# Attention, routed experts and a gated MLP in one kernel: turns moved among products, a last step in halves, register reads moved

## The chip, the cores and the metric

One core of one Trainium2 chip runs the whole program. The metric is the device time of one execution in microseconds, lower is better; the times shown are medians over several executions.

## The reference

Three stages over 3072 tokens of 512 features, all fp32:

```
y[:, t] = scale * q_t @ state_t,  state_t = gamma * state_{t-1} + k_t v_t^T      # linear attention, 4 x 8 heads of 64
e = argmax(x @ w_gate);  h = relu(x @ w1[e]);  out = gate_w * sigmoid(x @ w_output_gate)[e] * (h @ w2[e])   # 8 experts, 512 -> 1024 -> 512
xn = x / rms(x) * rms_g;  g = xn @ w_gate;  result = (g * sigmoid(g) * (xn @ w_val)) @ w_out                 # MLP, 512 -> 1536 -> 512
```

## The kernel before, in words

Every engine has its own program, written out by hand, and they meet in counting semaphores: `then_inc` at the end of an instruction, `wait_ge` in front of one. Nothing plans the order; it is the order of the calls. In loops over tiles and blocks a wait compares with a value computed from the loop's counter in the engine's registers.

Large products run in three parts: an operand is split into a high part (`...h`, fp32r, written by ScalarE) and a low part (`...l`, the rest, by VectorE), and high times high, high times low and low times high are summed in one bank of 128x512. So every weight and every activation passes ScalarE first and VectorE second.

Stage 1, attention: 24 units of 128 tokens. Each unit's rows are scattered by an indirect DMA to the rows of their expert.

Stage 2, experts: tiles of 128 rows of one expert. Tiles 0 and 1 (`LEAD`) are written out; 2 to 21 run in a loop, 22 and 23 (`SURE - 2`, `SURE - 1`) are written out since the first work for the MLP lies around them, and from 24 (`SURE`) on, loops run a tile where a flag `real` in memory says that it exists; with this data tiles 24 to 28 do. On TensorE a tile `a` (`expert_tile`) is: `up(a, at, 0)` and `up(a, at, 1)`, 12 products each, with a half of the hidden row block each; `turn_hidden`, four turns (transposes through TensorE) of the first half of `hid`, then `turn_rows(a + 1)`, four turns of the next tile's rows `xg`, then four of the second half of `hid`; `down_tile`, 24 products. ScalarE: `tile_result` of the tile before, then three copies of weights where the next expert's are being split (`EARLY`, `HELD_EARLY`), `relu` of half 0, the store of the result, `relu` of half 1, `turned_hi_parts` (`hidh` half 0, `xgh` of the next tile by `rows_hi`, `hidh` half 1) and one more copy of weights. VectorE follows with `w1l`/`w2l`, `hidl`, `xgl`, `hidl`. Each expert's weights are 8 pieces of 128x1024; one tile splits the four of w1, the next the four of w2. GpSimd fetches the next tile's rows by an indirect DMA into `xg` once `tile_turned` says that it is free. The turned halves of `hid` go to banks HT0 and HT1, the rows to XG_T.

Stage 3, MLP: 6 blocks of 512 tokens, 12 inner steps of 128 hidden columns each (`NF`). On TensorE a step is `gate_value(n, f)`, 24 products in two banks, then `down(n, f - 1)`, 12 products into four sums; `down(n, 11)` ends the block. Between them for each step: `gate_sigmoid` (ScalarE, `sig`), `gated` and `prod` (`hidden`, VectorE), `hidden_hi` (ScalarE, `hh`), `hidden_lo` (VectorE, `hl`), each one instruction on 128x512. Behind step 11 ScalarE and VectorE make the next block's `xh` and `xl` (`turned_hi`, `turned_lo`). For blocks 0 and 1 the normalised rows are turned by TensorE (`turn_xn`): for block 0 around tile 23, eight turns before it and eight behind it, for block 1 inside block 0's last step; for the later blocks by DMAs and VectorE. In front of block 0 TensorE reads `runs` and `extra` from memory (`value_load`), and `real` flags one by one.

## Time and profile before

| what | value |
|---|---|
| median of 3 executions | 1116.9 us (1116.73 to 1118.97) |
| the profiled execution | 1117.19 us, span of its instructions 1115.4 us |
| TensorE busy (PE), weight loads (PEld) | 1093.2 us (98%), 908.0 us (81%) |
| VectorE (DVE), ScalarE (ACT), GpSimd (POOL) | 441.2 us (40%), 377.8 us (34%), 176.9 us (16%) |
| chain of waits that ended last | PE 92%, DVE 3%, DMA 2%, issue 2%, ACT 1% |
| granted TensorE clock | 1.0 over the span |
| stages | attention to about 145 us, experts to about 515 us, MLP to the end |

Busy time counts an instruction from its start to its end; products of TensorE overlap, so 0.389 us of one product's duration stands for a pitch of 0.227 us from start to start. "issue" as a releaser means that the engine waited for nothing that the profile shows. Line numbers are those of the kernel before.

### The profile page before, as it was taken

Reading aid. Unit: us, or ns where it says so; the run is one execution under the profiler, and the core shown is the slowest. Engines: PE = TensorE matmul, PEld = TensorE weight load, DVE = VectorE, ACT = ScalarE, POOL = GpSimd, SP = SyncE. Lnnn points to the kernel's source line nnn. Section 1 sums busy time; section 2 is a strip of 40 time slices with the busy share of each in tenths; the row PEclk is TensorE's granted clock in tenths of the full one; section 3 lists DMA queues with packets and bytes.
Section 4 is the critical chain, followed back from the end, with each engine's and each line's share of the span. In section 5 each row is a group of like instructions: output and inputs, shape, how many; then the busy total and the mean of one; then the engine's idle time right before and its main releaser. Section 6 shows DMA issues by size and latency. Waiting matters only on the chain.

```text
span 1115.4 us, 20314 instructions
## 1 busy us (share of the span) xinstructions
PE 1093.2 (98%) x6307; PEld 908.0 (81%) x6308; DVE 441.2 (40%) x868; ACT 377.8 (34%) x613; POOL 176.9 (16%) x245
## 2 busy tenths in 40 slices
PE   7999999999999999999999999999999999999998
PEld 6888888888888888787888888788878878887886
DVE  4777767332414425432433333423333242333222
ACT  3545435343525446432224231231133122212112
POOL 2444423322221201000000300200030011001000
PEclk9999999999999999999999999999999999999999
DMA  9999816434445533422201210111021001101001
GB/s 216 243 252 240 245 61 211 148 113 122 113 122 168 172 122 133 153 76 97 63 6 34 76 35 4 47 28 38 0 75 26 12 38 38 38 0 38 1 1 38
DMA packets 114068, 101.52 MB, mean 91 GB/s; under 512 B 81856, under 2 KB 87392, under 8 KB 114016
## 3 DMA queue, kind: packets, MB, share of 16 engines
q1 hardware_dynamic: 98752, 66.07, 22.2%
q0 software_dynamic: 8832, 26.81, 7.7%
q10 hardware_dynamic: 6432, 7.96, 2.0%
q8 instruction: 31, 0.51, 0.2%
q14 instruction: 21, 0.17, 0.1%
HBM read 76.41 MB, written 20.22 MB: 87 GB/s over the span
## 4 chain that ended last, share of the span: by engine, by line
PE 92%; DVE 3%; DMA 2%; issue 2%; ACT 1%; POOL 0%; SPq 0%; POOLq 0%; ACTq 0%; DVEq 0%
PE bank L720 14%; PE bank L722 14%; PE bank L721 14%; PE banks L644 14%; PE bank L617 14%; PE banks L720 3%; PE banks L722 3%; PE banks L721 3%; PE bank L528 2%; PE banks L514 2%; PE bank L558 1%; DMA x_rows<-x_out,slot_idx 1%; PE banks L632 1%; PE bank L608 1%; PE bank L632 1%
## 5 line engine op out<-in xcount | busy, mean ns | idle before, releaser
L1397 DVE TENSOR_TENSOR gated<-bank,sig 128x512 f32<-128x512 f32 x72 | 49.8, 692 | 344.1 <-ACT sig L1011 344.1
L1011 ACT ACTIVATE sig<-bank 128x512 f32<-128x512 f32 x72 | 43.1, 598 | 328.9 <-PE bank L722 328.9
L720 PE MATMUL bank<-xh,w1h 128*128 128x512 f32 x384 | 149.4, 389 | 0.0
L721 PE MATMUL bank<-xl,w1h 128*128 128x512 f32 x384 | 149.4, 389 | 0.0
L722 PE MATMUL bank<-xh,w1l 128*128 128x512 f32 x384 | 149.4, 389 | 0.0
L721 PEld LDWEIGHTS bank<-xl,w1h 128*128 128x128 f32 x384 | 72.1, 188 | 15.0
L722 PEld LDWEIGHTS bank<-xh,w1l 128*128 128x128 f32 x384 | 72.1, 188 | 15.0
L720 PEld LDWEIGHTS bank<-xh,w1h 128*128 128x128 f32 x384 | 72.1, 188 | 14.9
L1018 ACT ACTIVATE hh<-prod 128x512 fp32r<-128x512 f32 x72 | 45.5, 632 | 110.7 <-DVE prod L1401 110.7
L1163 DVE TENSOR_TENSOR hidl<-bank,hidh 128x512 fp32r<-128x512 f32 x29 | 20.0, 691 | 131.8 <-ACT hidh L869 131.8
L1406 DVE TENSOR_TENSOR hl<-prod,hh 128x512 fp32r<-128x512 f32 x72 | 49.9, 692 | 54.2 <-ACT hh L1018 54.2
L1598 POOL DMA_INDIRECT out_rows<-x_out,cur_idx x10 | 10.1, 1007 | 380.4 <-ACT x_out L1025 290.0
L644 PE MATMUL banks<-w2h,hidh 128*128 (+1 forms) x232 | 64.8, 401 | 0.4
L617 PE MATMUL bank<-w1h,xgh 128*128 (+1 forms) x232 | 62.7, 392 | 1.3 <-issue 1.3
L1128 DVE TENSOR_TENSOR w1l<-stage,w1h 128x1024 f32 (+1 forms) x40 | 48.1, 1232 | 39.7 <-ACT w1h L821 39.7
L644 PE MATMUL banks<-w2h,hidl 128*128 (+1 forms) x232 | 62.2, 390 | 0.0
L644 PE MATMUL banks<-w2l,hidh 128*128 (+1 forms) x232 | 62.2, 390 | 0.0
L617 PE MATMUL bank<-w1h,xgl 128*128 (+1 forms) x232 | 62.2, 390 | 0.0
L617 PE MATMUL bank<-w1l,xgh 128*128 (+1 forms) x232 | 62.0, 389 | 0.0
L852 ACT ACTIVATE hid<-bank 128x512 f32<-128x512 f32 x58 | 34.4, 594 | 79.9 <-PE bank L617 79.9
L1503 POOL DMA_INDIRECT xg<-x_rows,cur_idx x28 | 28.6, 1022 | 206.4 <-PE bank L608 204.7
L720 PE MATMUL banks<-w2h,hh 128*128 128x512 f32 x144 | 56.8, 394 | 4.4 <-DVE hl L1406 4.4
(243 smaller groups left out, 2130.6 us busy)
## 6 DMA issues: line engine op xcount, KB each, us to landing
stage<-in_moe_w SPq DMA_DIRECT2D x64, 512.0 KB, 5.6
expert_rows<-tile_o ACTq DMA_DIRECT2D x29, 256.0 KB
q_raw<-in_q SPq DMA_DIRECT2D x24, 256.0 KB, 6.0
k_raw<-in_k SPq DMA_DIRECT2D x24, 256.0 KB, 6.5
v_raw<-in_v SPq DMA_DIRECT2D x24, 256.0 KB, 4.6
stage<-stage SPq DMA_DIRECT2D x64, 64.0 KB, 2.0
stage<-in_moe_w_out SPq DMA_DIRECT2D x6, 512.0 KB, 4.1
stage<-in_moe_w_gate SPq DMA_DIRECT2D x5, 512.0 KB, 5.4
```

The source lines that it names most:

```text
L617: mm = pe.matmul(bank[(UP0, UP1)[g]][:, :], x[:, i, :], wt[:, ds(at + (i * FE + g * 512), 512)], start=(n == 0), stop=(n == len(terms) - 1))
L644: mm = pe.matmul(bank[DOWN][:, :], x[:, f, :], wt[:, ds(at + f * D, D)], start=(f == 0 and x is hidh and wt is w2h), stop=(f == KE - 1 and ...
L720: pe.matmul(out_ap, lh, rh, start=first, stop=False)
L721: pe.matmul(out_ap, lh, rl, start=False, stop=False)
L722: return pe.matmul(out_ap, ll, rh, start=False, stop=last)
L852: nc.scalar.activation(hid[:, g * 512:(g + 1) * 512], bank[(UP0, UP1)[g]][:, :], ACT.Relu)\
L1011: nc.scalar.activation(sig[:], bank[GV[f % 2][0]][:, :], ACT.Sigmoid).then_inc(s["sig_done"], 1)
L1018: nc.scalar.activation(hh[:, f % 2, :], prod[:], ACT.Copy).then_inc(s["hid_hi"], 1)
L1128: nc.vector.tensor_tensor(into[:, ds(at, PIECE)], stage[:, i % STAGE, :], hi[:, ds(at, PIECE)].bitcast(F32), ALU.subtract).then_inc(s["lo_ ...
L1397: v3.tensor_tensor(gated[:], bank[GV[f % 2][0]][:, :], sig[:], ALU.mult).then_inc(s["gated_done"], 1)
L1406: v3.tensor_tensor(hl[:, f % 2, :], prod[:], hh[:, f % 2, :].bitcast(F32), ALU.subtract)\
L1503: nc.gpsimd.indirect_dma_start(xg[:].bitcast(U32), None, x_dram, bass.IndirectOffsetOnAxis(cur_idx[:, 0:1], 0))\
```

## The change

The change has six parts.

- A tile's turns on TensorE: `turn_hidden(a, 0)` stands in the middle of `up(a, at, 1)`, behind six of its products (`between`); `turn_hidden(a, 1)` in `down_tile`, behind the first four products; `turn_rows(a + 1)` between the two halves of `down_tile`.
- ScalarE and VectorE follow that order: `hidh` half 0, `relu` half 1, `hidh` half 1, `xgh`; `hidl`, `hidl`, `xgl`.
- Step 11 of each MLP block runs on VectorE as gate(0), product(0), gate(1), hl(0), product(1), hl(1), each on 256 of the 512 tokens, on ScalarE as one sigmoid and two copies for `hh`. A block counts 13 in the semaphores of these (`STEPS`). `down(n, 11)` waits for the second half before its third sum.
- TensorE's reads of `runs`, `extra` and `real[LIKELY]` move to places around tiles 22 and 23.
- `hidden_hi` waits for `down_done` before `prod_done`; it was the other way round.
- In block 0 the first products into bank XG_T wait for `tileT_lo` of the last tile.

```diff
 F2 = 1536
 NF = F2 // P
+STEPS = NF + 1
...
+        def halves(f):
+            return range(2 if f == NF - 1 else 1)
+
+        def step_no(n, f, half=0):
+            return STEPS * n + f + half
+
+        def tokens_of(f, half):
+            return slice(half * 2 * P, (half + 1) * 2 * P) if f == NF - 1 else slice(0, BLK * P)
...
-            def up(a, at, g):
+            def up(a, at, g, between=None):
                 if not (isinstance(a, int) and a == 0):
                     pe.wait_ge(s["relu_done"], 2 * a - 1 + g)
                 terms = [(x, wt, i) for x, wt in ((xgh, w1h), (xgh, w1l), (xgl, w1h)) for i in range(KD)]
                 for n, (x, wt, i) in enumerate(terms):
+                    if between and n == len(terms) // 2:
+                        between()
                     mm = pe.matmul(bank[(UP0, UP1)[g]][:, :], x[:, i, :], wt[:, ds(at + (i * FE + g * 512), 512)],
                                    start=(n == 0), stop=(n == len(terms) - 1))
                 mm.then_inc(s["up_done"], 1)
-            def turn_hidden(a):
-
-                first = isinstance(a, int) and a == 0
+            def turn_hidden(a, g):
+
+                pe.wait_ge(s["relu_done"], 2 * a + g + 1)
+                if not (isinstance(a, int) and a == 0):
+                    pe.wait_ge(s["hTl"], 2 * a - 1 + g)
+                for i in range(4):
+                    f = 4 * g + i
+                    mm = pe.transpose(quad((HT0, HT1)[g])[:, i, :], hid[:, f * P:(f + 1) * P], ident)
+                mm.then_inc(s["h_turned"], 1)
+
+            def down_tile(a, at):
+
+                if not (isinstance(a, int) and a == 0):
+                    pe.wait_ge(s["tile_out"], a)
                 for g in range(2):
                     if g:
                         turn_rows(a + 1)
-                    pe.wait_ge(s["relu_done"], 2 * a + g + 1)
-                    if not first:
-                        pe.wait_ge(s["hTl"], 2 * a - 1 + g)
-                    for i in range(4):
-                        f = 4 * g + i
-                        mm = pe.transpose(quad((HT0, HT1)[g])[:, i, :], hid[:, f * P:(f + 1) * P], ident)
-                    mm.then_inc(s["h_turned"], 1)
-
-            def down_tile(a, at):
-
-                if not (isinstance(a, int) and a == 0):
-                    pe.wait_ge(s["tile_out"], a)
-                for g in range(2):
                     for x, wt in ((hidh, w2h), (hidh, w2l), (hidl, w2h)):
+                        if not g and x is hidh and wt is w2l:
+                            turn_hidden(a, 1)
                         if wt is w2h:
                             pe.wait_ge(s["hTh" if x is hidh else "hTl"], 2 * a + g + 1)
                         for f in range(4 * g, 4 * g + 4):
...
                 run = pe.value_load(run_of[0:1, ds(a, 1)], min_val=0, max_val=EXPERTS - 1)
                 pe.wait_ge(s["tileT_lo"], a + 1)
                 pe.wait_ge(s["lo_done"], RUN * run + PER)
-                for g in range(2):
-                    up(a, at, g)
-                turn_hidden(a)
+                up(a, at, 0)
+                up(a, at, 1, lambda: turn_hidden(a, 0))
                 pe.wait_ge(s["lo_done"], RUN * run + RUN)
                 down_tile(a, at)
...
             gate_logits(last)
             pe.wait_ge(s["x_out"], last)
             turn_x(last)
-            up(0, 0, 1)
+            up(0, 0, 1, lambda: turn_hidden(0, 0))
             ranks(last)
-            turn_hidden(0)
             pe.wait_ge(s["xT_out"], UNITS)
             down_tile(0, 0)
             for a in range(1, LEAD):
                 pe.wait_ge(s["tileT_lo"], a + 1)
-                for g in range(2):
-                    up(a, 0, g)
-                turn_hidden(a)
+                up(a, 0, 0)
+                up(a, 0, 1, lambda: turn_hidden(a, 0))
                 down_tile(a, 0)
             def turn_xn(n, halves):
...
             pe.wait_ge(s["control_ready"], 1)
             with pe.Fori(LEAD, SURE - 2) as a:
                 expert_tile(a)
+            runs = pe.value_load(flags[0:1, 0:1], min_val=0, max_val=EXPERTS - 2) + 2
             expert_tile(SURE - 2)
+            extra = pe.value_load(flags[0:1, 2:3], min_val=0, max_val=TILES - SURE)
             turn_xn(0, [0])
+            unlikely = pe.value_load(real[0:1, LIKELY:LIKELY + 1], min_val=0, max_val=1)
             expert_tile(SURE - 1)
             pe.wait_ge(s["xl_ready"], 2)
             turn_xn(0, [1])
-            runs = pe.value_load(flags[0:1, 0:1], min_val=0, max_val=EXPERTS - 2) + 2
-            extra = pe.value_load(flags[0:1, 2:3], min_val=0, max_val=TILES - SURE)
-
             def tile_if_real(a):
                 with pe.If(pe.value_load(real[0:1, ds(a, 1)], min_val=0, max_val=1)):
                     expert_tile(a)
             with pe.Fori(SURE, LIKELY) as a:
                 tile_if_real(a)
-            with pe.If(pe.value_load(real[0:1, LIKELY:LIKELY + 1], min_val=0, max_val=1)):
+            with pe.If(unlikely):
                 with pe.Fori(LIKELY, TILES) as a:
                     tile_if_real(a)
...
                         pe.wait_ge(s["early_done"], 2)
             def gate_value(n, f):
-                g = NF * n + f
-                if f >= 2 or not (isinstance(n, int) and n == 0):
-                    pe.wait_ge(s["prod_done"], g - 1)
+                if f >= 2:
+                    pe.wait_ge(s["prod_done"], step_no(n, f - 1))
+                elif not (isinstance(n, int) and n == 0):
+                    pe.wait_ge(s["prod_done"], step_no(n, 0) - (0 if f else 2))
                 for m in range(2):
+                    if isinstance(n, int) and n == 0 and GV[f % 2][m] == XG_T and f < 2:
+                        pe.wait_ge(s["tileT_lo"], extra + SURE + 1)
+                        pe.sem_inc(s["stood"], 1)
                     weights_ready(n, m, f)
                     for i in range(KD):
                         if f == 0 and m == 0:
...
                 mm.then_inc(s["gv_done"], 1)
             def down(n, f):
-                g = NF * n + f
-                pe.wait_ge(s["hid_lo"], g + 1)
+                pe.wait_ge(s["hid_lo"], step_no(n, f) + 1)
                 weights_ready(n, 2, f)
                 if f == 0 and isinstance(n, int) and n == 0:
                     pe.wait_ge(s["tile_out"], extra + SURE)
...
                 elif f == 0:
                     pe.wait_ge(s["sum_out"], BLK * n)
                 for t in range(BLK):
+                    if f == NF - 1 and t == BLK // 2:
+                        pe.wait_ge(s["hid_lo"], step_no(n, f, 1) + 1)
                     col = slice(t * P, (t + 1) * P)
                     mm = three(bank[SUM[t]][:, :], (hh[:, f % 2, col], hl[:, f % 2, col]), out_parts(f),
                                f == 0, f == NF - 1)
...
                 for f in range(NF):
                     gate_value(n, f)
                     if f == NF - 1 and turns:
-                        pe.wait_ge(s["prod_done"], NF * n + NF - 1)
+                        pe.wait_ge(s["prod_done"], step_no(n, NF - 1))
                         turn_xn(n + 1, [0])
                     if f:
                         down(n, f - 1)
                 if turns:
-                    pe.wait_ge(s["prod_done"], NF * (n + 1))
+                    pe.wait_ge(s["prod_done"], step_no(n + 1, 0))
                     turn_xn(n + 1, [1])
                 down(n, NF - 1)
...
                 for g in range(2):
                     if g:
-                        rows_hi(a + 1)
+                        relu(a, 1)
                     act.wait_ge(s["h_turned"], 2 * a + g + 1)
                     if g == 0 and not (isinstance(a, int) and a < 1):
                         act.wait_ge(s["tiles_done"], a + 1)
                     nc.scalar.activation(hidh[:, 4 * g:4 * g + 4, :], quad((HT0, HT1)[g]), ACT.Copy).then_inc(s["hTh"], 1)
+
+                rows_hi(a + 1)
             def tile_result(a):
                 act.wait_ge(s["tiles_done"], a + 2)
...
                     split_run_hi(turn, to, range(PER, HELD_EARLY))
                 relu(a, 0)
                 store_tile(a - 1)
-                relu(a, 1)
                 turned_hi_parts(a)
                 with act.If(is_go):
                     split_run_hi(turn, to, range(EARLY, PER))
...
             evacuate_yT(UNITS - 1)
             relu(0, 0)
             evacuate_x(UNITS - 1)
-            relu(0, 1)
             turned_hi_parts(0)
             for a in range(1, LEAD):
                 tile_result(a - 1)
                 relu(a, 0)
-                relu(a, 1)
                 turned_hi_parts(a)
                 put_tile(a - 1, (a - 1) * P)
             exps()
...
             def gate_sigmoid(n, f):
-                g = NF * n + f
-                act.wait_ge(s["gv_done"], g + 1)
-                if not (isinstance(n, int) and g < 1):
-                    act.wait_ge(s["gated_done"], g)
+                act.wait_ge(s["gv_done"], NF * n + f + 1)
+                if f or not isinstance(n, int) or n:
+                    act.wait_ge(s["gated_done"], step_no(n, f))
                 nc.scalar.activation(sig[:], bank[GV[f % 2][0]][:, :], ACT.Sigmoid).then_inc(s["sig_done"], 1)
             def hidden_hi(n, f):
                 g = NF * n + f
-                act.wait_ge(s["prod_done"], g + 1)
                 if not (isinstance(n, int) and g < 2):
                     act.wait_ge(s["down_done"], BLK * (g - 1))
-                nc.scalar.activation(hh[:, f % 2, :], prod[:], ACT.Copy).then_inc(s["hid_hi"], 1)
+                for half in halves(f):
+                    part = tokens_of(f, half)
+                    act.wait_ge(s["prod_done"], step_no(n, f, half) + 1)
+                    nc.scalar.activation(hh[:, f % 2, part], prod[:, part], ACT.Copy).then_inc(s["hid_hi"], 1)
             def sums_out(n):
                 for t in range(BLK):
...
                   .then_inc(s["hTl"], 1)
             def turned_lo_parts(a):
-                for g in range(2):
-                    if g:
-                        rows_lo(a + 1)
-                    hidden_lo_part(a, g)
+                hidden_lo_part(a, 0)
+                hidden_lo_part(a, 1)
+                rows_lo(a + 1)
             choose(UNITS - 2)
             rows_lo(0)
...
                     split_run_lo(RUN * (run + 1), to, range(HELD_EARLY, RUN))
             for a in range(1, LEAD):
+                hidden_lo_part(a, 1)
                 rows_lo(a + 1)
-                hidden_lo_part(a, 1)
             gates_of_rows()
             for i in range(PRE_A, PRE):
                 split_pre_lo(i)
...
                          HALF + (i % PER) * PIECE)
-            def hidden(n, f):
-
-                g = NF * n + f
-                dve.wait_ge(s["sig_done"], g + 1)
-                v3.tensor_tensor(gated[:], bank[GV[f % 2][0]][:, :], sig[:], ALU.mult).then_inc(s["gated_done"], 1)
-                dve.wait_ge(s["gated_done"], g + 1)
-                if not (isinstance(n, int) and g < 1):
-                    dve.wait_ge(s["hid_lo"], g)
-                v3.tensor_tensor(prod[:], bank[GV[f % 2][1]][:, :], gated[:], ALU.mult).then_inc(s["prod_done"], 1)
-
-            def hidden_lo(n, f):
-                g = NF * n + f
-                dve.wait_ge(s["hid_hi"], g + 1)
-                v3.tensor_tensor(hl[:, f % 2, :], prod[:], hh[:, f % 2, :].bitcast(F32), ALU.subtract)\
+            def gate(n, f, half):
+                part = tokens_of(f, half)
+                dve.wait_ge(s["sig_done"], NF * n + f + 1)
+                v3.tensor_tensor(gated[:, part], bank[GV[f % 2][0]][:, part], sig[:, part], ALU.mult)\
+                  .then_inc(s["gated_done"], 1)
+
+            def product(n, f, half):
+                part = tokens_of(f, half)
+                dve.wait_ge(s["gated_done"], step_no(n, f, half) + 1)
+                if f or not isinstance(n, int) or n:
+                    dve.wait_ge(s["hid_lo"], step_no(n, f))
+                v3.tensor_tensor(prod[:, part], bank[GV[f % 2][1]][:, part], gated[:, part], ALU.mult)\
+                  .then_inc(s["prod_done"], 1)
+
+            def hidden_lo(n, f, half):
+                part = tokens_of(f, half)
+                dve.wait_ge(s["hid_hi"], step_no(n, f, half) + 1)
+                v3.tensor_tensor(hl[:, f % 2, part], prod[:, part], hh[:, f % 2, part].bitcast(F32), ALU.subtract)\
                   .then_inc(s["hid_lo"], 1)
             def ffn_block(n):
                 final = isinstance(n, int) and n == NBLK - 1
                 for f in range(NF):
-                    hidden(n, f)
-                    hidden_lo(n, f)
+                    gate(n, f, 0)
+                    product(n, f, 0)
+                    if f == NF - 1:
+                        gate(n, f, 1)
+                    hidden_lo(n, f, 0)
+                    if f == NF - 1:
+                        product(n, f, 1)
+                        hidden_lo(n, f, 1)
                     if isinstance(n, int) and n == 0 and f < RUN:
                         split_rest(f)
                     if final:
```

## Rows read from the trace of the kernel before

**Rows 1.** The page: busy time and share of each engine.
```profile
PE 1093.2 (98%) x6307; PEld 908.0 (81%) x6308; DVE 441.2 (40%) x868; ACT 377.8 (34%) x613; POOL 176.9 (16%) x245
```

**Rows 2.** Waits, longest in total: us, times, longest; releaser behind the arrow.
```profile
PE banks L720 <- DVE hl L1406: 4.4, 5, 0.9
...
PEld banks L644 <- issue: 6.0, 27, 0.2
```

**Rows 3.** Timeline, an ordinary tile: start, duration (us), instructions, count.
```profile
210.68 1.07 PE L617 MATMUL bank<-w1h,xgh 128*128 x4
...
216.13 0.60 PE L632 MATMUL bank<-con,hid 128*128 128x128 f32 x4
216.56 0.60 PE L608 MATMUL bank<-con,xg 128*128 128x128 f32 x4
...
217.64 1.16 PE L644 MATMUL banks<-w2h,hidh 128*128 x4
...
223.17 1.07 PE L617 MATMUL bank<-w1h,xgh 128*128 x4
```

**Rows 4.** Timeline of ScalarE in the same tile; brackets: idle before, releaser.
```profile
216.32 0.60 ACT L852 ACTIVATE hid<-bank 128x512 f32<-128x512 f32 x1 [2.13 <-PE bank L617]
216.82 0.59 ACT L869 ACTIVATE hidh<-bank 128x512 fp32r<-128x512 f32 x1
```

**Rows 5.** Timeline of TensorE, tiles 23 and 24 and the bursts before.
```profile
435.90 0.60 PE L689 MATMUL bank<-con,x_out 128*128 128x128 f32 x4
...
436.69 1.17 PE L617 MATMUL bank<-w1h,xgh 128*128 x4
...
442.23 0.60 PE L632 MATMUL bank<-con,hid 128*128 128x128 f32 x4
...
451.50 0.49 PE L617 MATMUL bank<-w1h,xgh 128*128 x1 [0.98 <-issue]
```

**Rows 6.** Timeline, start of a tile that splits weights.
```profile
198.13 1.07 PE L617 MATMUL bank<-w1h,xgh 128*128 x4
...
201.79 0.57 ACT L852 ACTIVATE hid<-bank 128x512 f32<-128x512 f32 x1
```

**Rows 7.** Timeline, tiles 23 and 24: relu on ScalarE, a late weight load.
```profile
441.34 0.60 ACT L852 ACTIVATE hid<-bank 128x512 f32<-128x512 f32 x1
...
454.53 0.60 ACT L852 ACTIVATE hid<-bank 128x512 f32<-128x512 f32 x1
...
445.70 0.76 PEld L644 LDWEIGHTS banks<-w2h,hidl 128*128 128x128 f32 x4 [0.30 <-DVE hidl L1163]
```

**Rows 8.** Timeline, tile 2: its first products, VectorE's first `hidl`.
```profile
173.00 1.19 PE L617 MATMUL bank<-w1h,xgh 128*128 x4 [0.34 <-issue]
...
180.48 0.68 DVE L1163 TENSOR_TENSOR hidl<-bank,hidh 128x512 fp32r<-128x512 f32 x1
```

**Rows 9.** Timeline, end of MLP block 2, all engines.
```profile
808.10 0.39 PE L720 MATMUL banks<-w2h,hh 128*128 128x512 f32 x1
...
808.30 0.60 ACT L1011 ACTIVATE sig<-bank 128x512 f32<-128x512 f32 x1 [5.36 <-PE bank L722]
...
808.93 0.69 DVE L1397 TENSOR_TENSOR gated<-bank,sig 128x512 f32<-128x512 f32 x1 [5.27 <-ACT sig L1011]
...
810.46 0.63 ACT L1018 ACTIVATE hh<-prod 128x512 fp32r<-128x512 f32 x1 [1.57 <-DVE prod L1401]
...
811.12 0.69 DVE L1406 TENSOR_TENSOR hl<-prod,hh 128x512 fp32r<-128x512 f32 x1 [0.78 <-ACT hh L1018]
...
811.87 0.50 PE L720 MATMUL banks<-w2h,hh 128*128 128x512 f32 x1 [0.89 <-DVE hl L1406]
...
814.77 0.39 PE L720 MATMUL bank<-xh,g01h 128*128 128x512 f32 x1
```

**Rows 10.** Groups by line and shape: count, busy us, mean ns.
```profile
L1080 DVE COPY state<-bank 128x256 f32<-128x256 f32 x20 | 8.5, 425 | 14.4 <-PE bank L544 14.4
...
L821 ACT ACTIVATE w1h<-stage 128x1024 f32 x28 | 28.2, 1057 | 0.0
```

More of the change, by code:

```diff
@@ L619, in up @@
                 mm.then_inc(s["up_done"], 1)
-            def turn_hidden(a):
-                first = isinstance(a, int) and a == 0
-                for g in range(2):
-                    if g:
-                        turn_rows(a + 1)
-                    pe.wait_ge(s["relu_done"], 2 * a + g + 1)
-                    if not first:
-                        pe.wait_ge(s["hTl"], 2 * a - 1 + g)
-                    for i in range(4):
-                        f = 4 * g + i
-                        mm = pe.transpose(quad((HT0, HT1)[g])[:, i, :], hid[:, f * P:(f + 1) * P], ident)
-                    mm.then_inc(s["h_turned"], 1)
+            def turn_hidden(a, g):
[6 more added lines that the diff above has]
+                mm.then_inc(s["h_turned"], 1)
             def down_tile(a, at):
@@ L639, in down_tile @@
                 for g in range(2):
+                    if g:
+                        turn_rows(a + 1)
                     for x, wt in ((hidh, w2h), (hidh, w2l), (hidl, w2h)):
+                        if not g and x is hidh and wt is w2l:
+                            turn_hidden(a, 1)
                         if wt is w2h:
@@ L1166, in turned_lo_parts @@
             def turned_lo_parts(a):
-                for g in range(2):
-                    if g:
-                        rows_lo(a + 1)
-                    hidden_lo_part(a, g)
+                hidden_lo_part(a, 0)
+                hidden_lo_part(a, 1)
+                rows_lo(a + 1)
             choose(UNITS - 2)
```

## The prediction

> **What bounds the kernel now.** I read the busy table first: TensorE works 98% of the span [rows 1], so a change can only pay where TensorE waits or runs something it need not. The list of waits comes next. It has TensorE's products L720 waiting for VectorE's `hl` 5 times, 4.4 us in all, and its weight loads L644 held 27 times by "issue", 6.0 us in all [rows 2]. The first stands at the end of MLP blocks, the second once in nearly every expert tile; these are the two places that the change rearranges. So I read one of each in the timeline, to see what each really costs, because a pipeline that has run empty loses more than the idle time shows.
>
> An ordinary expert tile takes 223.17 - 210.68 = 12.49 us. Its 24 up products take 5.45, which is 0.227 each, so 48 products are 10.90 and 1.59 is left for the 12 turns (transposes). Four turns take 0.43, or 0.108 each [rows 3]. A burst of eight turns ends after 0.79, and the 24 products behind it take 5.54 instead of 5.45, so the burst costs 0.88: eight times 0.108 and 0.02 for getting back to products [rows 5]. By that measure twelve turns should cost 1.32; the tile's real wait before the down products is 1.59 - 1.32 = 0.27 us.
>
> An MLP block ends with down step 10 (from 808.10) and down step 11 (ends at 814.77): 6.67 us for 24 products worth 5.45, so 1.22 are lost [rows 9]. It happens in blocks 1 to 5; in block 0 turns of the next block's rows cover it, which is why the list counts 5.
>
> **MLP, last step in halves.** The chain today: sigmoid at 808.30, gated 808.93, prod behind it, `hh` 810.46, `hl` 811.12, TensorE goes on at 811.87 [rows 9]. Step 10's twelve products end at 808.10 + 2.72 = 810.82. Half tiles: no 128x256 product of two tensors is in the trace. From below it can't be under half of 0.69, 0.35; from above it isn't over the whole one, 0.69. The nearest row is a 128x256 copy at 0.425, and on ScalarE the slope from 128x512 (0.63) to 128x1024 (1.057) puts 256 columns at 0.42 [rows 9, 10]; I take 0.42 for both. Then gate(0) runs 808.93 to 809.35, product(0) from 809.38, hh(0) from 809.88 (0.08 after the product, where the whole one shows up to 0.1), hl(0) from 810.33 to 810.75, seen at 810.80. TensorE wants the weights one product, 0.23, before the products, at 810.59. So it is 0.2 late, and with what an emptied pipeline loses I leave 0.27 of the 1.22. The second half: gate(1) runs while ScalarE has hh(0); product(1) 810.67, hh(1) 811.15, hl(1) 811.60 to 812.02. It is wanted six products later, about 812.15, and is in time. The gain is 0.95 a block, 4.75 for five. With half tiles at 0.35 all 1.22 go (6.1); at 0.55 the first half is 0.5 later, 0.45 a block is left (2.3); at 0.69 nothing. What comes behind on VectorE and ScalarE is the next block's `xh` and `xl`, now about 0.5 later by the clock while TensorE wants them 1 us sooner; operations like these take up to 0.69 each, and TensorE asks for one per three products, 0.68, so they stay ahead by about half a microsecond. In block 0 the turns cover both halves.
>
> The Trainium skill ("VectorE: DVE Perf Modes", the TRN2 errata) says that a fixed latency is paid per instruction, and advises tiles of at least 512 elements; its fp32 tensor_tensor formula gives 0.424 us for 256 columns and 0.691 for 512. The trace agrees on the second (0.69). By the rule halving adds 0.16 to every operation in total work; what would speak against the change is the case where this fixed part falls on the path a second time, which is rival 2.
>
> **Expert tiles, turns among products.** The 12 turns stay, but in three bursts, each with products behind. The wait of 0.27 before the down products goes: the first half of `hidden` is now turned six products (1.36) ahead of them, its `hidh` needs about 0.25 + 0.60. What is late next? For burst 2: relu(a,1) starts 0.19 after the up products, takes 0.60 [rows 4], 0.05 until seen, 0.84 in all; four products cover 0.91. That is just enough. For the next tile's rows: turned half-way through down, 12 products (2.72) cover `xgh` and `xgl`, about 0.25 + 0.60 + 0.70. The indirect DMA behind them starts 3 us later and still has a whole period of 12.5 until its rows are turned. Getting back to products is paid three times: from 0.02 each (the burst of eight) to 0.09 (the loss seen in the products behind it, with nothing given back) [rows 5]. Three bursts of four cost 3 x (0.43 + 0.02) = 1.35 up to 1.56; I take 0.05 each, nearer the first: 1.44 against 1.59, less what rounding hides, so 0.17 saved where nothing new waits.
>
> Something new waits in many tiles. In a tile in which the next expert's weights are split, ScalarE puts three 128x1024 copies before relu(a,0). Tile start 198.13, relu(a,0) ends 201.79 + 0.57 = 202.36, i.e. 4.23 into the tile [rows 6]. Before it was wanted after 24 products (5.45), now after 18 (4.08), and 0.05 later it is seen: 0.20 waited. There are 14 such tiles: 28 such copies of w1h, four a tile [rows 10], and as many of w2h in the tiles behind those. In 13 of them -0.03 results. The 14th, tile 23, has MLP work on ScalarE in front: tile start 436.69, relu(23,0) ends 441.94 [rows 5, 7], wanted at 440.86, so 1.13 waited; on the other side its weight loads now wait 0.30 for `hidl` [rows 7], which that covers: -0.7 net. In tile 2 VectorE still splits four late weights before hidl(2,0), which ends at 180.48 + 0.68 = 181.16 [rows 8]. It is wanted 32 products and two bursts into the tile, 8.2 after 173.00, less 0.23: 180.97. So VectorE sets that point, whatever tiles 0 and 1 gain, and I count 0 for tiles 0 to 2. The sum over 29 tiles: 12 ordinary x 0.17 = 2.0, 13 x -0.03 = -0.4, tile 23 -0.7: a gain of 0.9. Bounds: with getting back at 0.02 there are 26 x 0.09 more, 3.2 in all; with 0.09 it is -2.2, and with burst 2 late by another 0.1 as well, -4.8.
>
> **TensorE's reads.** Before tile 24 TensorE idles 0.98 by "issue": five register reads behind eight short turns [rows 5]. Two of them move to where products queue. ScalarE limits what that brings: relu(24,0) ends 454.53 + 0.60 = 455.13 [rows 7]; the burst that needs it is due at 451.50 + 4.17 = 455.67, so at most about 0.5 can be gained before the burst waits for it. I take 0.4, and 0.1 for the `unlikely` read gone from before tile 27 (half of the 0.2 that one of five reads is of 0.98). Moved reads stand behind products or turns: tile 23 now has three behind its turns where it had two, which could cost up to 0.3. Lower bound -0.3, upper 0.9. The added waits in block 0 ask for things done some 10 us earlier and have only products behind them: nothing.
>
> **Sum.** 4.75 + 0.9 + 0.5 = 6.15. The profiled execution took 1117.19 (span 1115.4), so 1111.0; it lies 0.3 above the median of the three runs, 1116.9. I say 1110.8.
>
> **Rivals.** 1, getting back to products is free. For it: a burst of eight shows 0.02 net; against it: 0.09 lost behind it, and short bursts mean more borders. Then an ordinary tile gains 0.27 and the splitting ones 0.07; 12 x 0.27 + 13 x 0.07 - 0.6 = 3.6 from the experts instead of 0.9: 1108.1, and with the MLP wait gone whole 1106.7. The Trainium skill ("TensorE: Matmul & The Clock Gate", Back-to-back issue gap) has TensorE pull weight loads ahead of products in flight, which would favour this.
>
> 2, the halves are as long as the whole, because the fixed part stands on the path again and each wait with a register sum adds its own. For it: `hh` starts up to 0.1 late behind such a wait; against it: the copy at 0.425. The MLP gains nothing, 1115.5.
>
> 3, slower than before: bursts expose TensorE's own waits. In front of every burst stand two waits on computed values, behind the rows' turns a third kind. Today three of them behind one burst come with 0.27 [rows 2, 3], 0.09 each. If no product hides them, seven a tile cost 0.63 and 26 tiles 16: 1127. It turns slower than before once it exceeds 6.15 / 26 = 0.24 a tile. For it: the 0.22 a tile called "issue"; against it: turns with two such waits in front of them follow at 0.43 per four without a gap [rows 3], and most bursts now come out of a run of products.
>
> **How the numbers follow.** Forecast 0.62, rival 1 0.20, rival 2 0.08, rival 3 0.05, something else 0.05. The likeliest one's own bounds are about 1107.5 to 1114. The range takes in rival 1, down to 1106.5, and up to 1114.3 part of a failed MLP half. 0.2%, what a measurement tells from no change here, is 2.2 us: below 1114.7 is faster. Forecast, rival 1 and half of the rest give 0.86 faster; rival 2 is mostly "same", 0.09; slower 0.05.
>
> **What would show it.** The five waits of L720 for `hl` shrink to 0.3 or less each, and the copies of half width on VectorE and ScalarE take about 0.42. The 0.22 "issue" waits before L644's first product go. Tiles without splitting last about 12.3, those with it 12.5 with a new wait of the first hidden turns (L632) for relu L852, 1.1 in tile 23; tile 2 waits for `hidl`. The 0.98 before tile 24 is about halved. The prediction is wrong if half-width operations take 0.55 or more, if turns in the middle of products wait in ordinary tiles too, or if the span falls by over 9 us.

## The result and the profile after

The changed kernel is slower: 1127.27 us (median of 4, 1126.36 to 1128.53) against 1116.82 for the kernel before on the same chip, ratio 1.0088 with a 95% interval of 1.0072 to 1.0104. Forecast was 1110.8, range 1106.5 to 1114.3. The profiled execution took 1126.71, its span is 1124.9.

Two lines of the page of after; the first answers to [rows 1]. The second is the chain of waits by engine, where TensorE fell from 92% to 83% and work of the other engines' queues came in.

```profile
PE 1090.6 (97%) x6307; PEld 902.9 (80%) x6308; DVE 448.5 (40%) x886; ACT 388.1 (34%) x619; POOL 181.5 (16%) x245
...
PE 83%; ACTq 4%; issue 4%; DVE 4%; ACT 2%; DMA 1%; DVEq 0%; POOL 0%; SPq 0%; POOLq 0%
```

The waits of after (us in all, times, longest), answering to [rows 2]:

```profile
PE bank L640 <- ACT hid L866: 15.8, 14, 2.1
...
PE banks L656 <- DVE hidl L1177: 1.8, 2, 1.5
...
ACT tile_o L891 <- issue: 34.8, 12, 5.1
```

Both lines of [rows 2] are gone. In their place the turns of `hid` (L640 now) wait for ScalarE's relu (L866 now) 15.8 us in 14 tiles. The third line belongs to ScalarE: 12 times `tile_o`, its first work of a tile, is held by "issue", that is by nothing that the profile shows. In the trace of before this stood once, 2.2 us in front of tile 24; the other 26 waits of `tile_o` there are put down to TensorE.

From start to start on TensorE the tiles last as follows; the stage from tile 1 to the MLP's first product took 356.66 us before and 371.21 after (+14.55), the MLP 598.8 and 594.9 (-3.9); tile 1 starts 1.1 earlier, which does not show in every kernel with turns (159.90 in one, 159.91 before).

| tiles | before | after | sum of the difference |
|---|---|---|---|
| 9 ordinary of tiles 5 to 21 | 12.49 to 12.55 | 12.26 to 12.30 | -2.2 |
| 5 that split w1 (3, 7, 11, 15, 18) | 12.5 | 13.08 (tile 3: 13.42) | +3.2 |
| 5 that split w2 (4, 8, 12, 16, 19) | 12.5 | 14.05 to 14.13 | +7.8 |
| 1, 2 | 13.09, 12.63 | 14.97, 12.88 | +2.1 |
| 22, 23, 24 | 13.29, 14.81, 12.61 | 13.22, 14.53, 13.04 | +0.1 |
| 25, 26 (split w1, w2) | 12.54, 12.56 | 13.73, 14.71 | +3.3 |
| 27, 28 with the way into the MLP | 12.68, 14.68 | 12.43, 15.10 | +0.2 |

TensorE's timeline in an ordinary tile of after, where [rows 3] stood for before: 238.73 (not shown) - 226.46 = 12.27, no idle bracket anywhere. The burst of four turns takes 0.35, and the two products behind it 0.55 instead of 0.45, so 0.45 in all.

```profile
226.46 1.07 PE L629 MATMUL bank<-w1h,xgh 128*128 x4
...
230.09 0.62 PE L629 MATMUL bank<-w1l,xgh 128*128 x2
230.55 0.60 PE L640 MATMUL bank<-con,hid 128*128 128x128 f32 x4
230.90 0.71 PE L629 MATMUL bank<-w1l,xgh 128*128 x2
```

The same in a tile that splits w2, with ScalarE beside it (timeline of after; [rows 6] is its counterpart):

```profile
197.59 0.60 ACT L873 ACTIVATE xgh<-bank 128x512 fp32r<-128x512 f32 x1 [1.79 <-PE bank L618]
...
198.09 1.05 ACT L835 ACTIVATE w1h<-stage 128x1024 f32 x1
...
200.06 1.07 PE L629 MATMUL bank<-w1h,xgh 128*128 x4
...
201.86 0.60 ACT L891 ACTIVATE tile_o<-banks 128x512 f32<-128x512 f32 x1 [2.72 <-issue]
...
202.37 2.01 ACT L835 ACTIVATE w2h<-stage 128x1024 f32 x2
...
204.28 1.04 ACT L835 ACTIVATE w2h<-stage 128x1024 f32 x1
205.23 0.57 ACT L866 ACTIVATE hid<-bank 128x512 f32<-128x512 f32 x1
...
205.86 0.66 PE L640 MATMUL bank<-con,hid 128*128 128x128 f32 x4 [1.55 <-ACT hid L866]
```

The relu ends 5.74 into the tile (205.80 - 200.06), not 4.23. The copies before it last what they lasted; `tile_o` starts 1.80 after the tile. Read ScalarE upwards from it: 2.72 idle, and before that the last copy of weights (to 199.14), and before that `xgh`, which the new order makes at 197.59, 2.5 before the tile ends. The same stretch of ScalarE in the kernel before:

```profile
192.72 0.61 ACT L869 ACTIVATE hidh<-banks 128x512 fp32r<-128x512 f32 x1
193.20 1.09 ACT L821 ACTIVATE w1h<-stage 128x1024 f32 x1
198.43 0.60 ACT L875 ACTIVATE tile_o<-banks 128x512 f32<-128x512 f32 x1 [4.14 <-PE banks L644]
198.93 2.96 ACT L821 ACTIVATE w2h<-stage 128x1024 f32 x3
```

There ScalarE was through at 194.29 and had 4.14 us until TensorE's last products released it, 0.30 after the tile's start at 198.13. In the ordinary tiles of after (5 to 17) `tile_o` is late too, 0.83 to 1.07 into the tile, in tile 6 2.68 behind ScalarE's last work, although the profile puts most of these waits down to TensorE. What ScalarE does in these microseconds has no row: the four register reads (`value_load` of `go`, `held`, `run_of`, `next_at`) and the branches of the next tile.

The end of MLP block 2 in after, [rows 9] being before's:

```profile
821.92 0.39 PE L729 MATMUL banks<-w2h,hh 128*128 128x512 f32 x1
822.12 0.60 ACT L1023 ACTIVATE sig<-bank 128x512 f32<-128x512 f32 x1 [5.45 <-PE bank L731]
...
822.75 0.42 DVE L1409 TENSOR_TENSOR gated<-bank,sig 128x256 f32<-128x256 f32 x1 [5.36 <-ACT sig L1023]
...
823.67 0.42 ACT L1032 ACTIVATE hh<-prod 128x256 fp32r<-128x256 f32 x1 [0.95 <-DVE prod L1417]
...
824.12 0.42 DVE L1423 TENSOR_TENSOR hl<-prod,hh 128x256 fp32r<-128x256 f32 x1 [0.15 <-ACT hh L1032]
...
824.64 0.47 PE L729 MATMUL banks<-w2h,hh 128*128 128x512 f32 x1
...
827.50 0.39 PE L729 MATMUL bank<-xh,g01h 128*128 128x512 f32 x1
```

24 products in 5.58 us (827.50 - 821.92) instead of 6.67: 1.09 gained. And the way into the MLP, first the timeline, then the windows (columns: busy time and instructions of each engine, the granted clock as a share of full speed, DMA share, GB/s):

```profile
530.00 0.67 PE L729 MATMUL bank<-xh,g01h 128*128 128x512 f32 x1 [2.54 <-issue]
530.46 0.63 PE L730 MATMUL bank<-xl,g01h 128*128 128x512 f32 x1
530.89 0.63 PE L731 MATMUL bank<-xh,g01l 128*128 128x512 f32 x1
...
530.00:533.00 3.00, 3.00 (x7) 2.38 (x8) 0.00 (x0) 0.60 (x1) 0.00 (x0) 0.52 0.23 87
```

After 2.54 us without a product (2.0 before) the granted clock is 0.52, its lower level of 1.2 GHz: products follow at 0.43 instead of 0.227 us, eight of them, some 1.6 us. The MLP of the kernel with halves and reads, whose clock stayed at full speed there, takes 593.3 us against the 594.9 here.

### The profile page after: what moved, and what is told of

Read it like the earlier page. It is cut to its first block, busy times and chain, and to the rows that moved or that the text cites. A ratio compares the mean times of both kernels' runs of the same rounds, so it can differ in the third digit from the quotient of the medians.

```text
span 1124.9 us, 20454 instructions
## 1 busy us (share of the span) xinstructions
PE 1090.6 (97%) x6307; PEld 902.9 (80%) x6308; DVE 448.5 (40%) x886; ACT 388.1 (34%) x619; POOL 181.5 (16%) x245
## 4 chain that ended last, share of the span: by engine, by line
PE 83%; ACTq 4%; issue 4%; DVE 4%; ACT 2%; DMA 1%; DVEq 0%; POOL 0%; SPq 0%; POOLq 0%
PE bank L729 15%; PE bank L731 15%; PE bank L730 15%; PE banks L656 10%; PE bank L629 8%; PE banks L729 3%; PE banks L730 3%; PE banks L731 3%; PE bank L538 2%; PE banks L524 2%; PE bank L568 1%; PE bank L640 1%; PE bank L618 1%; PE banks L517 1%; PE banks L640 1%
## 5 line engine op out<-in xcount | busy, mean ns | idle before, releaser
L1409 DVE TENSOR_TENSOR gated<-bank,sig 128x512 f32<-128x512 f32 (+1 forms) x78 | 50.7, 650 | 339.6 <-ACT sig L1023 339.6
L1032 ACT ACTIVATE hh<-prod 128x512 fp32r<-128x512 f32 (+1 forms) x78 | 46.7, 599 | 109.9 <-DVE prod L1417 108.9
L1423 DVE TENSOR_TENSOR hl<-prod,hh 128x512 fp32r<-128x512 f32 (+1 forms) x78 | 50.9, 652 | 51.2 <-ACT hh L1032 51.2
L629 PE MATMUL bank<-w1l,xgh 128*128 (+1 forms) x232 | 69.5, 401 | 0.0
L656 PE MATMUL banks<-w2l,hidh 128*128 (+1 forms) x232 | 65.2, 403 | 0.0
L1142 DVE TENSOR_TENSOR w2l<-stage,w2h 128x1024 f32 (+1 forms) x40 | 47.5, 1223 | 27.1 <-ACT w2h L835 27.1
L730 PE MATMUL banks<-w2l,hh 128*128 128x512 f32 x144 | 56.2, 390 | 0.0
```

Of the source, the lines that this page charges most:

```text
L629: mm = pe.matmul(bank[(UP0, UP1)[g]][:, :], x[:, i, :], wt[:, ds(at + (i * FE + g * 512), 512)], start=(n == 0), stop=(n == len(terms) - 1))
L656: mm = pe.matmul(bank[DOWN][:, :], x[:, f, :], wt[:, ds(at + f * D, D)], start=(f == 0 and x is hidh and wt is w2h), stop=(f == KE - 1 and ...
L730: pe.matmul(out_ap, lh, rl, start=False, stop=False)
L1032: nc.scalar.activation(hh[:, f % 2, part], prod[:, part], ACT.Copy).then_inc(s["hid_hi"], 1)
L1142: nc.vector.tensor_tensor(into[:, ds(at, PIECE)], stage[:, i % STAGE, :], hi[:, ds(at, PIECE)].bitcast(F32), ALU.subtract).then_inc(s["lo_ ...
L1409: v3.tensor_tensor(gated[:, part], bank[GV[f % 2][0]][:, part], sig[:, part], ALU.mult)\
```

## The experiments

**The three parts by themselves**, each put into the kernel before. The halves:

```
+  for half in halves(f): ... activation(hh[:, f % 2, part], prod[:, part])     # and gate, product, hidden_lo on VectorE
```

> Only the last MLP step in halves; turns and reads as before. Theory (the halves work, the loss of the whole change lies in the expert tiles): about 1.1 us less at the end of each of blocks 1 to 5, 1111.3 us, tiles as before (12.5 us). Rival (the MLP is shorter in the changed kernel only because it starts in another state, the halves themselves are worth nothing): 1116.8 us.

1112.06 us, ratio 0.9953 [0.9936, 0.9969], about 5.2 us less, near the 1111.3 expected. The MLP takes 595.0 against 598.8, and no wait of a product for `hl` is left. These 3.8 us are the gain less some 1.6, since in this profile too the clock was at its lower level (0.50) at the MLP's start; with the clock at full speed the MLP in halves takes 593.3, 5.5 less, or 1.1 a block.

The turns:

```
-  for g in range(2): up(a, at, g)
-  turn_hidden(a)
+  up(a, at, 0)
+  up(a, at, 1, lambda: turn_hidden(a, 0))     # and ScalarE's and VectorE's order
```

> Only the turns among the products, with the order of ScalarE and VectorE that goes with them. Theory (ScalarE's register reads for the next tile, 2.7 us, had idle time to hide in and now stand behind the late xgh copy, so relu of half 0 is late wherever three weight copies stand in front of it): ordinary tiles 12.3, tiles that split w1 13.1, those that split w2 14.1 us; 1131 to 1133 us. Rival (the loss comes from the three parts together, above all from the moved reads): 1118 or less.

1134.67, ratio 1.0161 [1.0144, 1.0178]: the whole loss is here, 18 us, which is 1.7 more than the upper end expected. The tiles came as expected and as in after: 12.27, 13.08, 14.06 to 14.14. The expectation did not work out tiles 1, 23 and 26, which take 1.9, 1.0 and 2.9 more than before.

The reads:

```
+  runs = pe.value_load(...); expert_tile(SURE - 2); extra = pe.value_load(...); turn_xn(0, [0])
+  unlikely = pe.value_load(...); expert_tile(SURE - 1)
```

> Only TensorE's reads moved. Theory: 0.3 to 0.6 us less before tile 24, nothing elsewhere, 1116.4 us, same. Rival (moved reads make TensorE late or slow its clock at the start of the MLP): idle time before the first MLP product over 2.5 us and half clock for some 4 us behind it, 1118.5 us.

1116.16, ratio 0.9992 [0.9982, 1.0002], not told from no change. Its timeline before tile 24, where [rows 5] had 0.98 idle:

```profile
449.79 0.60 PE L689 MATMUL bank<-con,more_rows 128*128 128x128 f32 x4
450.14 1.17 PE L617 MATMUL bank<-w1h,xgh 128*128 x4
```

No idle is left; tile 23 takes 13.55 instead of 14.81, tile 27 12.49 instead of 12.68: 1.45 us gained where 0.5 was predicted and at most 0.6 expected. In this profile the clock then fell at the MLP's start, behind an idle time of 2.03 that is no longer than before's (2.02), and took most of it back (MLP 600.2 against 598.8):

```profile
514.90:518.00 3.10, 3.10 (x8) 2.42 (x9) 0.00 (x0) 1.28 (x1) 0.00 (x0) 0.54 0.16 59
```

Executions can also be compared at the same clock. Where the granted clock of the whole execution was 1.0, the medians are 1115.1 (4 of 10) against 1116.6 before (12 of 19); where it was 0.998, 1116.8 against 1117.8. So the reads bring some 0.9 to 1.5 us, and it is hidden in the median because more of the executions had the lower value.

**ScalarE's reads one tile ahead**, in after. The theory: `tile_o` is late since the reads now stand behind a late `xgh`.

```
 def turned_hi_parts(a):
     ...                                          # hidh 0, relu 1, hidh 1
+    read_ahead(a + 1)                            # the four numbers into registers kept to the next tile
     rows_hi(a + 1)
```

> The changed kernel, but ScalarE reads a tile's four numbers one tile ahead, before it waits for the turned rows, where it is idle for 1.8 us. Theory (those reads are the cause): ScalarE's result copy starts 0.3 us after the tile's end again, w1 and w2 tiles last 12.4 to 12.7 us, tile 23 still waits 1.1 us for its relu; 1111 to 1114 us. Rival (the late weight copy and the late xgh themselves fill ScalarE): w2 tiles stay at 13.5 us or more, 1122 us or more.

1113.72, ratio to before 0.9973 [0.9963, 0.9982], within what was expected: 13.5 us less than after (12.8 by the ratios) by four reads moved. ScalarE in the tile that splits w2 (start 199.48):

```profile
197.02 0.60 ACT L873 ACTIVATE xgh<-bank 128x512 fp32r<-128x512 f32 x1 [1.77 <-PE bank L618]
197.51 1.05 ACT L835 ACTIVATE w1h<-stage 128x1024 f32 x1
199.78 0.60 ACT L893 ACTIVATE tile_o<-banks 128x512 f32<-128x512 f32 x1 [1.21 <-PE banks L656]
200.29 2.96 ACT L835 ACTIVATE w2h<-stage 128x1024 f32 x3
203.15 0.58 ACT L866 ACTIVATE hid<-bank 128x512 f32<-128x512 f32 x1
```

`xgh` and the copy stand where they stood in after, but `tile_o` is 0.30 behind the tile's start again, released by TensorE, and the relu ends at 203.73, 4.25 into it, as the prediction had taken it. Splitting tiles take 12.51 to 12.56, except 18, 19 and 26 (12.99, 12.62, 13.38), where the relu is in time as well and what holds the tile was not followed; the wait of L640 for `hid` is down to one, 0.9 in tile 23.

**Twice the reads**, in after and, as its control, in before:

```
-  is_go, is_held, turn, to = numbers or tile_numbers(a)
+  is_go, is_held, turn, to, go_late, held_late, turn_late, to_late = numbers or both_numbers(a)
```

> The changed kernel with ScalarE's four register reads of a tile made twice (8 instead of 4, same place, the second set steers the late weight copy). Theory (the reads behind the late xgh copy set the pace of the tiles that split weights): 1.5 to 2.2 us more in each of the 14 splitting tiles, ordinary tiles still 12.3, 1148 to 1158 us. Rival (the order of ScalarE's copies is the cause, reads are hidden): 1127 to 1129 us.

1180.39, ratio 1.0544 [1.0526, 1.0562], beyond what either theory gave (1148 to 1158 at most). ScalarE's `tile_o`:

```profile
191.54 0.60 ACT L891 ACTIVATE tile_o<-banks 128x512 f32<-128x512 f32 x1 [5.12 <-issue]
...
209.30 0.60 ACT L891 ACTIVATE tile_o<-banks 128x512 f32<-128x512 f32 x1 [4.85 <-issue]
```

These are tiles 3 and 4; in after they waited 3.00 and 2.72, so four more reads cost 2.1, some 0.53 us each. Splitting tiles grow to 15.1 to 18.9, by more than those 2.1, and the granted clock of the whole execution is 0.977 (0.998 in after). In tile 4 the two can be told apart: the burst stands 7.92 into the tile instead of 5.80, 2.1 later, and the other 1.5 of its 17.76 - 14.11 come from the burst on, at the lower clock (0.90 over this tile, 1.00 in after).

> The kernel before with the same eight reads instead of four. Theory: its 4 to 5 us of idle time ahead of each result copy covers them, 1117 to 1118 us, every tile 12.5. Rival (reads cost TensorE something wherever they stand): over 1125 us.

1118.19, ratio 0.9997 [0.9987, 1.0006]. In the order of before the same four reads are free. They do not quite fit into the 4.14 us, though; the tile that splits w2 shows it:

```profile
198.25 0.60 ACT L875 ACTIVATE tile_o<-banks 128x512 f32<-128x512 f32 x1 [4.73 <-PE banks L644]
...
201.62 0.58 ACT L852 ACTIVATE hid<-bank 128x512 f32<-128x512 f32 x1
```

`tile_o` starts 0.85 into this tile (start 197.40) instead of 0.30, and the relu ends at 4.80 instead of 4.23. TensorE wants it at 5.45 in this order, so nothing waits. In the changed order, which wants it at 4.1, the same relu would be late. It is the place of the reads, and how early the relu is wanted, that makes them cost something, not their number alone.

**The other remedy: `xgh` early again**, in after. The next tile's rows are turned beside the second half of `hid`, behind the first four down products, and ScalarE and VectorE take them first.

```
 if not g and x is hidh and wt is w2l:
+    turn_rows(a + 1)
     turn_hidden(a, 1)
```

> The changed kernel, but the next tile's rows are turned in one burst with the second half of hid, behind the first four down products; ScalarE and VectorE make xgh and xgl before hidh and hidl of half 1, as the kernel before does. ScalarE's last copy is then over about 4 us before the tile's end, and its reads are covered without being moved. Theory: w1 and w2 tiles 12.5, ordinary tiles 12.2 to 12.3, tile 23 still with its wait, 1111 to 1113 us. Rival (turns among products lose wherever weights are split, since relu of half 0 stands behind three copies): w1 and w2 tiles over 13 us, 1120 us or more.

1113.7, ratio 0.9964 [0.9954, 0.9975], 0.7 above what was expected; splitting tiles up to 19 take 12.50 to 12.62, ordinary ones 12.27. ScalarE is through at 208.12 in the tile that begins at 198.27, and `tile_o` of the next is released by TensorE with 3.10 to spare:

```profile
206.09 0.60 ACT L872 ACTIVATE xgh<-bank 128x512 fp32r<-128x512 f32 x1 [0.85 <-PE bank L618]
...
207.06 1.06 ACT L834 ACTIVATE w2h<-stage 128x1024 f32 x1
211.22 0.60 ACT L889 ACTIVATE tile_o<-banks 128x512 f32<-128x512 f32 x1 [3.10 <-PE banks L655]
```

Two remedies that share nothing but the distance between ScalarE's last work of a tile and its next `tile_o` bring nearly the same: 12.8 and 13.9 us of after's time by the ratios.

**Both remedies, and tile 1.**

> Both remedies at once: the next tile's rows turned together with the second half of hid, and ScalarE's numbers read one tile ahead. Each alone gave 1113.7, with splitting tiles at 12.50 to 12.62 and ordinary ones at 12.27. Theory (either remedy alone already takes ScalarE's relu off TensorE's way; what is left is elsewhere): the tiles stay as they are within 0.1, tile 23 at about 14.3, and the time is 1112.5 to 1114. Rival (each remedy alone leaves splitting tiles 0.25 above the ordinary 12.27 because ScalarE is still just late): splitting tiles go to 12.3, 13 of them by 0.25, and the time is about 1110.5.

1112.33, ratio 0.9958 [0.9945, 0.9971], an interval that overlaps with each remedy's own. The tiles up to 21 are unchanged (12.50 to 12.54 splitting, 12.27 ordinary), so what is left is not ScalarE's reads. Tile 1 remained: TensorE in after and, below, with tile 1 alone put back in the order of before in the kernel with the early reads.

> The kernel after with ScalarE's four numbers read one tile ahead, and tile 1 alone in the order of before on all engines (three bursts behind its 24 up products, ScalarE relu, relu, hidh, xgh, hidh). In the new order tile 1 took 14.98 us, 1.54 of it a wait of its third group of down products for VectorE's hidl, which stands behind the routing arithmetic until 168.25. In the order of before that hidl is wanted about 1.3 us later, and tile 1 took 13.1. Theory (what is left of the loss in tile 1 is VectorE's routing, met earlier by the new order): tile 1 falls to 13.1 to 13.6 and the kernel goes from 1113.7 to 1111.9 to 1112.4. Rival (the routing chain sets when TensorE goes on whatever the order, since tile 2 needs its rows and tables too): tile 1 loses less than 0.5 of it or tile 2 grows by as much, and the time stays at 1113.3 to 1113.9.

```profile
168.70 1.19 PE L656 MATMUL banks<-w2h,hidl 128*128 128x512 f32 x4 [1.54 <-DVE hidl L1177]
```

```profile
167.97 0.66 PE L618 MATMUL bank<-con,xg 128*128 128x128 f32 x4 [2.57 <-DMA xg<-x_rows,cur_idx]
```

Tile 1 went from 14.98 to 15.50 and tile 2 from 12.88 to 12.43, together 27.93 against 27.86: the rival's case by the tiles. The wait for VectorE's `hidl` (behind its routing arithmetic) is replaced by one for the rows of tile 2, whose indices come out of the same arithmetic. GpSimd's timeline shows it, first in this kernel, then in the kernel before:

```profile
163.58 0.18 POOL L1532 COPY cur_idx<-row_idx 128x1 uint32<-128x1 uint32 x1 [8.69 <-DVE row_idx L1237]
```

```profile
161.65 0.18 POOL L1497 COPY cur_idx<-row_idx 128x1 uint32<-128x1 uint32 x1 [6.64 <-DVE row_idx L1212]
```

The arithmetic stands behind VectorE's work of tile 0, which now ends with `xgl` of rows that are turned half-way through that tile's down products; so it is 1.9 later by the two traces' time, 2.5 counted from the start of tile 1, and its results with it. The time, 1112.12, ratio 0.9959 [0.9946, 0.9971], lies where the theory had it and not the rival. But it differs from 1113.72 by no more than the intervals allow, and in this profile the clock stayed at full speed at the MLP's start, which it did not in that of the early reads; so the tiles decide, and not the time.

**Halves and reads without the turns**, the parts that paid.

```
   before + halves + moved reads of TensorE; order of the expert tiles as in before
```

> Halves and moved reads without the turns: what is left of the change if its losing part is dropped. Theory: the two gains add up, tile 23 ends 1.2 us sooner, 1110.5 to 1111.5 us. Rival (the gains overlap): 1112 us, as the halves alone.

1110.62 (1109.92 to 1110.94), ratio 0.9926 [0.9910, 0.9943], as expected: the fastest of all that ran, and 16.7 us below after by the medians (18 by the ratios). In all four executions the granted clock was 1.0. The reordered waits of `hidden_hi` and of block 0's first products were never run by themselves; they are in the kernels with halves and with turns.

## Why the prediction was wrong

**The step that failed** is "Tile start 198.13, relu(a,0) ends 201.79 + 0.57 = 202.36, i.e. 4.23 into the tile [rows 6]. Before it was wanted after 24 products (5.45), now after 18 (4.08), and 0.05 later it is seen: 0.20 waited." The demand side was right; the supply side was carried over from before as a constant. But 4.23 held only because `tile_o` began with TensorE's release, and that only because ScalarE had 4.14 us to read its registers in. The change itself moves `xgh` behind the second `hidh` and half of the down products, in an ordinary tile to 9.81 instead of 6.61, and eats this time. After an ordinary tile the 2.7 us of reads and branches then end 0.83 into the next tile, after one that splits w1, with its late copy (1.05), 1.80 into it. So relu(a,0) comes 0.55 or 1.5 later, and 13.08 and 14.05 to 14.13 follow instead of 12.5. Where the prediction had 13 splitting tiles lose 0.4 together, the twelve of them other than 22 cost 14.3. Moving the reads alone, or `xgh` alone, brings the relu back to 4.2; doubling the reads in before costs nothing. With the early reads that is shown for tiles 3 to 25; tile 26 keeps 0.8 of its loss there (13.38) with its relu in time, from something else. With the rows early it is shown for tiles 3 to 23. The prediction asked what is late next for TensorE's bursts and for VectorE's `xgl`, but not what ScalarE does behind `xgh`; its trace had the sign, since "issue" stood before ScalarE's `tile_o` too, once, for 2.2 us.

**What was right.** An ordinary tile: 12.3 predicted, 12.26 to 12.30. Tile 23: a burst 1.13 late was predicted. With the early reads it starts 5.31 into the tile where 4.17 was reckoned, 1.14 late. In after it is 1.32 late; that the profile calls 1.13 of it idle (it counts from the end of the last product) is a coincidence. The loss of that tile was put at 0.7 and is 0.97 (14.81 to 15.78) in the kernel with turns alone. The half-width operations: 0.42 each, predicted 0.42. The five waits of products for `hl` are gone; up to 0.3 is left at the weight loads.

**What was mis-sized.** The halves: 0.95 a block, measured 1.09, 5.45 in all instead of 4.75. Getting back to products: 0.05 taken for each burst, 0.02 measured (a burst costs 0.45, of which 0.43 are the turns), so an ordinary tile gains 0.25 (12.27 against 12.52 on average) where 0.17 was taken; the prediction's own terms, 1.59 - 1.44, give 0.15. The reads: 0.5 predicted, 1.45 by the tiles of the kernel with reads alone. "ScalarE limits what that brings" was worked out for the turned order; in the order of before relu(24,0) is wanted later. In the changed kernel, against turns alone, tiles 23 and 24 together gain 0.63 for 0.4, and tile 24 does wait 0.40 for its relu; but tile 26 gains 0.70 where the `unlikely` read was put at 0.1. Tiles 0 to 2, "counted 0": tile 1 costs 1.9, since VectorE's routing arithmetic begins 2.5 later, counted from the start of tile 0 (12.65 instead of 10.12), behind the late `xgl` of tile 0, and a `hidl` wanted earlier stands behind it.

**The rivals.** Rival 3 gave 1127, and 1127.27 came, but its mechanism is refuted: it wanted 0.6 more in every tile, and the ordinary ones got 0.2 shorter without an idle bracket. Its number is a coincidence. Rival 2 is refuted by the 0.42. Rival 1 would have had ordinary tiles gain 0.27, the forecast 0.17; 0.25 is nearer rival 1, so getting back to products is almost free here. Its time failed on the same relu as the forecast.

**The sum anew**, from the profiles: halves -5.45; tiles +14.55, which holds the reads' gain; the clock at the MLP's start +1.6; tile 1's earlier start -1.1; together +9.6, where the profiled executions differ by 1126.71 - 1117.19 = 9.52.

**What stays open.** Even with ScalarE out of the way the turned order does not beat the old one: from tile 1 to the MLP it takes 357.9 us with the early reads and 357.0 with both remedies, halves and reads alone 355.8. Nine ordinary tiles give 2.2, while tiles 1, 23 and the last ones, with a branch in front of each, and 0.5 to 1.1 more idle before the MLP take more than that. Which of these could be had back was not tried.

## What to carry to other kernels

When a change makes a point of demand earlier, recompute the supplier's whole path, its register reads and branches too: they have no rows, and show only as idle time that is put down to whatever ended it. An engine's idle time before a wait is slack only as long as nothing else is moved into it; ask of each operation that comes later what stands behind it in its own program. A number read in one order ("4.23 into the tile") is a result of that order, not a property of the work.

## What the hardware showed

ScalarE's register reads cost about 0.53 us each (2.1 for four more of them), and the four with their branches 2.7 us ahead of an operation that nothing else holds. Half-width tensor operations took 0.420 to 0.425 us on VectorE and 0.418 on ScalarE, 0.69 and 0.63 at full width; these are the groups that answer to [rows 10]:

```profile
L1423 DVE TENSOR_TENSOR hl<-prod,hh 128x256 fp32r<-128x256 f32 x12 | 5.1, 425 | 3.9 <-ACT hh L1032 3.9
...
L1032 ACT ACTIVATE hh<-prod 128x256 fp32r<-128x256 f32 x12 | 5.0, 418 | 10.8 <-DVE prod L1417 9.8 <-PE banks L731 1.0
```

The same idle time of TensorE was followed by the clock's lower level in one profile and not in another, all at the MLP's start. Behind 1.97 to 2.03 us the clock fell in two profiles (halves alone 0.50, reads alone 0.54) and stayed in three (before, halves and reads, twice the reads in before); behind 2.52 to 2.55 it fell in three (after, turns alone, early reads) and stayed in one (tile 1 alone put back); behind 3.14 it fell with the rows early and stayed with both remedies. It varies between executions of one kernel as well: the kernel before had a granted clock of 1.0 over the whole in 12 of 19 executions and 0.998 in the others, with medians 1.1 us apart. In these eleven profiles 0.998 over the whole went with the fall at the MLP's start, and 1.0 with none. The fall is worth some 1.6 us, which is why single profiles of two kernels should not be compared at that place. The Trainium skill ("TensorE: Matmul & The Clock Gate", Part 1) says that the number of slow matmuls at a kernel's start varies from run to run. No run here shows that; what varies here is whether the clock falls in the middle of a kernel.
